# A fused attention and two-layer feed-forward kernel on one core: the up projections recast as Strassen block products

## Time and profile before

| | |
|---|---|
| median of 3 runs | 982.44 us (980.26 to 982.64) |
| the profiled execution | 981.53 us |
| its span in the trace | 979.7 us, mean granted TensorE clock 0.993 |
| PE busy | 956.1 us, 98% |
| DVE, ACT, POOL busy | 49%, 22%, 20% |

### The profile page before, as it was taken

How to read it: one execution, slowest core, us unless ns; L and a number is a source line. 1 busy time by engine, 2 the same in 40 slices (tenths; PEclk the granted TensorE clock), 3 DMA queues, 4 the chain that set the end, 5 groups by cost and what they waited for, 6 DMA issues and landing times.

```text
span 979.7 us, 14496 instructions
## 1 busy us (share of the span) xinstructions
PE 956.1 (98%) x5292; PEld 907.5 (93%) x5292; DVE 481.3 (49%) x895; ACT 219.0 (22%) x444; POOL 198.2 (20%) x211
## 2 busy tenths in 40 slices
PE   6999899999999999999999989999999999999998
PEld 5998899999999999999999968888888888889997
DVE  6776745634634634544555588343334334334332
ACT  4887642210200210110210011111012112111111
POOL 5679473000000000000028896000000000000000
PEclk9999899999999999999999989999999999999999
DMA  8897152000000000000013231010001001001001
GB/s 247 218 229 189 27 146 65 2 1 1 1 0 0 0 0 0 0 0 0 0 33 87 86 86 55 0 39 0 0 0 39 0 0 39 0 0 40 1 1 37
DMA packets 54065, 40.83 MB, mean 42 GB/s; under 512 B 21264, under 2 KB 44304, under 8 KB 54032
## 3 DMA queue, kind: packets, MB, share of 16 engines
q1 hardware_dynamic: 54032, 40.38, 14.9%
HBM read 35.65 MB, written 4.72 MB: 41 GB/s over the span
## 4 chain that ended last, share of the span: by engine, by line
PE 89%; POOL 3%; issue 3%; DMA 1%; DVE 1%; ACT 1%; SPq 0%; POOLq 0%; DVEq 0%; ACTq 0%
PE bank L558 29%; PE bank L559 29%; PE bank L560 29%; POOL probs L462 1%; DMA q_diag<-in_qT 1%; POOL half_sum L456 1%; PE bank L548 1%; PE bank L526 1%; PE bank L534 1%; DVE x_hi L911 0%; PE bank L554 0%; ACT probs L705 0%; POOL mask L429 0%; PE bank L517 0%; POOL ssum L287 0%
## 5 line engine op out<-in xcount | busy, mean ns | idle before, releaser
L558 PE MATMUL bank<-h_hi,wts 128*128 128x384 f32 (+2 forms) x608 | 216.5, 356 | 0.1
L559 PE MATMUL bank<-h_lo,wts 128*128 128x384 f32 (+2 forms) x608 | 215.6, 355 | 0.0
L560 PE MATMUL bank<-h_hi,wts 128*128 128x384 f32 (+2 forms) x608 | 215.1, 354 | 0.0
L558 PE MATMUL bank<-x_split_sb,wts 128*128 128x384 f32 x576 | 193.5, 336 | 0.0
L560 PE MATMUL bank<-x_split_sb,wts 128*128 128x384 f32 x576 | 193.2, 335 | 0.0
L559 PE MATMUL bank<-x_split_sb,wts 128*128 128x384 f32 x576 | 192.9, 335 | 0.0
L935 DVE TENSOR_TENSOR h_f<-h_f 128x464 f32<-128x464 f32 (+1 forms) x80 | 56.7, 709 | 144.1 <-ACT h_f L763 144.1
L558 PE MATMUL bank<-x_hi,wts 128*128 128x464 f32 (+1 forms) x320 | 120.4, 376 | 4.7 <-DVE x_lo L916 4.6
L558 PEld LDWEIGHTS bank<-h_hi,wts 128*128 128x128 f32 x608 | 114.2, 188 | 7.6 <-DVE h_lo L863 0.4
L559 PEld LDWEIGHTS bank<-h_lo,wts 128*128 128x128 f32 x608 | 114.1, 188 | 7.0
L560 PEld LDWEIGHTS bank<-h_hi,wts 128*128 128x128 f32 x608 | 114.2, 188 | 6.3
(11 more groups left out here) (63 smaller groups left out, 1029.3 us busy)
## 6 DMA issues: line engine op xcount, KB each, us to landing
k_sb<-in_kT SPq DMA_DIRECT2D x16, 288.0 KB, 4.0
q_diag<-in_qT SPq DMA_DIRECT2D x32, 144.0 KB, 4.5
v_odd<-in_v_odd SPq DMA_DIRECT2D x16, 256.0 KB, 2.9
v_even<-in_v_even SPq DMA_DIRECT2D x16, 256.0 KB, 3.2
raw<-in_w_in SPq DMA_DIRECT2D x16, 256.0 KB, 2.7
raw<-in_w_down SPq DMA_DIRECT2D x16, 256.0 KB, 2.6
out_T<-acts SPq DMA_DIRECT2D x16, 232.0 KB, 2.0
raw<-in_w_gate SPq DMA_DIRECT2D x12, 256.0 KB, 3.2
```

Source lines behind the costliest of these rows:

```text
L558: pe.matmul(ps, w_hi, v_hi, start=first, stop=False)
L559: pe.matmul(ps, w_hi, v_lo, start=False, stop=False)
L560: return pe.matmul(ps, w_lo, v_hi, start=False, stop=last)
```

## The change

**Shape of the work.** Tokens are taken in 3 pairs of 384-token tiles (768 tokens). There are six runs: the first layer for each pair, then the second layer for each pair. A run first does all its up products and keeps the hidden activations `h` in SBUF (up to 16 x 768 x 4 bytes per partition), then all its down products, chunk by chunk, for both halves of the pair.

**Up products.** A step takes a 2 by 2 arrangement: two blocks of 128 output features (gate and value of one chunk in the first layer, two chunks in the second), two halves of the 512 input features, two tiles of the pair. In place of 8 block products it makes 7 (`p1` to `p7`, Strassen's scheme in Winograd's form), each of 6 matmuls of 384 columns, on sums of weight blocks (S1 to S4) and sums of input blocks (T1 to T4). There are 12 steps in a run of the first layer, 8 in one of the second. PE's order in step u is p1, p7, p3 of step u-1, p6, p2, p4, p5.

**What goes with it.** The split weights are no longer kept: SP streams the raw weights for every run (three DMAs, 512 KB, a step; `load_w`), into two buffers in turn. POOL makes the four weight sums of step u+2 (`weight_sums`, 256 elements a partition each), ACT rounds 1024 and 768 elements a partition (`high1`, `high2`), DVE makes the rests of both (`low1`, `low2`). ACT copies three partial results out of PSUM (`c_t`, `c_p7`, `c_u`), DVE adds the others to them (c11, c21, c22), ACT, DVE and POOL form h from them (`gate_a`, `gate_b`, `silu_a`, `silu_b`, `h_a`, `h_b`; in the second layer ReLU and squares). The sums of squares for the next pair are seven POOL operations of 768 elements, in steps 1 to 7 of the first two runs. In the down part of a run each chunk has 24 matmuls; ACT rounds its weights and h (`down_high` 512 elements, `h_high` 768), POOL and DVE make the rests (`down_low`, `h_low`), and the input blocks of the next run are summed and split (four sums of 768 on DVE, seven roundings on ACT, seven rests on DVE), beginning at chunk 5 of a gated run that is followed by another and at chunk 1 otherwise; the first two steps' weight sums of the next run are made in chunks 2 and 3.

**Attention.** Its loops over batches are written out. The rounding of first-layer weights leaves it; two steps' weight sums, 14 sums of squares of 384 elements in groups 18 to 24 and 28 to 34, two mean squares with root and reciprocal (near groups 28 and 38), eight normalisings, and the blocks of the first pair (from group 34 on) come into it. The first up product follows the last slot.

The diff, cut to its core (a line of "..." marks what is left out):

```diff
+PW = 2 * NT
+PAIRS = TOKENS // PW
...
+UP_STEPS = [C1] * PAIRS + [C2 // 2] * PAIRS
+CHUNKS = [C1] * PAIRS + [C2] * PAIRS
+RUNS = 2 * PAIRS
+U0 = [sum(UP_STEPS[:n]) for n in range(RUNS + 1)]
+M0 = [sum(CHUNKS[:n]) for n in range(RUNS + 1)]
+B_BANKS = (3, 2, 0, 1)
...
+    def load_w(u):
+        if u >= 2:
+            sp.wait_ge(lo1_done, u - 1)
+            sp.wait_ge(lo2_done, u - 1)
+        r = max(n for n in range(RUNS) if U0[n] <= u)
+        s = u - U0[r]
+        one, two_ = ((w_gate, s), (w_val, s)) if first_layer(r) else ((w_in, 2 * s), (w_in, 2 * s + 1))
+        rows = [w.rearrange("(k p) f -> p k f", p=P)[:, :, n * P:(n + 1) * P] for w, n in (one, two_)]
+        to = w_in_sem[u % 2]
+        sp.dma_start(raw_part(u, RAW_A11, 2).rearrange("p (k f) -> p k f", k=KT), rows[0]).then_inc(to, 16)
+        sp.dma_start(two(raw_part(u, RAW_A21)), rows[1][:, 0:2, :]).then_inc(to, 16)
+        sp.dma_start(two(raw_part(u, RAW_A22)), rows[1][:, 2:4, :]).then_inc(to, 16)
...
+    for r in range(RUNS):
+        for u in range(U0[r] + (2 if r == 0 else 3), U0[r + 1] + 2):
+            if u < U0[RUNS]:
+                load_w(u)
+        for m in range(M0[r] + 2, M0[r + 1] + 2):
+            if m < M0[RUNS]:
+                load_d(m)
+        if r + 1 < RUNS:
+            load_w(U0[r + 1] + 2)
+        if not first_layer(r):
+            store(r, 0)
+            store(r, 1)
...
+    def weight_sum(u, i):
+        if i == 0:
+            pool.wait_ge(w_in_sem[u % 2], 48 * (u // 2 + 1))
+            nc.gpsimd.tensor_tensor(raw_part(u, RAW_S1), raw_part(u, RAW_A21), raw_part(u, RAW_A22),
+                                    ALU.add).then_inc(s_add, 1)
+        if i == 1:
+            nc.gpsimd.tensor_tensor(raw_part(u, RAW_S3), raw_part(u, RAW_A11), raw_part(u, RAW_A21),
+                                    ALU.subtract).then_inc(s_add, 1)
+        if i == 2:
+            pool.wait_ge(s_add, 4 * u + 1)
+            nc.gpsimd.tensor_tensor(raw_part(u, RAW_S2), raw_part(u, RAW_S1), raw_part(u, RAW_A11),
+                                    ALU.subtract).then_inc(s_add, 1)
+        if i == 3:
+            pool.wait_ge(s_add, 4 * u + 3)
+            nc.gpsimd.tensor_tensor(raw_part(u, RAW_S4), raw_part(u, RAW_A12), raw_part(u, RAW_S2),
+                                    ALU.subtract).then_inc(s_add, 1)
+    def weight_sums(u):
...
+    def h_a(u, r):
+        n = u - U0[r]
+        if first_layer(r):
+            pool.wait_ge(silu_a_done, u + 1)
+            pool.wait_ge(c21_done, u + 1)
+            nc.gpsimd.tensor_tensor(h_half(n, 0), ga[:], va[:], ALU.mult).then_inc(ha_done, 1)
...
+    def h_b(u, r):
+        n = u - U0[r]
+        if first_layer(r):
+            pool.wait_ge(silu_b_done, u + 1)
+            pool.wait_ge(c22_done, u + 1)
+            nc.gpsimd.tensor_tensor(h_half(n, 1), sbuf_b[:], vb[:], ALU.mult).then_inc(hb_done, 1)
...
+    for r in range(RUNS):
+        for u in range(U0[r], U0[r + 1]):
+            s = u - U0[r]
+            if s >= 1:
+                h_a(u - 1, r)
+            if u + 2 < U0[r + 1]:
+                weight_sums(u + 2)
+            if s >= 1:
+                h_b(u - 1, r)
+            if r + 1 < PAIRS and 1 <= s <= SQ_STEPS:
+                if s == 1 and r == 0:
+                    pool.wait_ge(o_out, 2 * GROUPS)
+                if s == 1 and r > 0:
+                    pool.wait_ge(norm_done, 2 * KT + KT * r)
+                square_step(nc.gpsimd, s - 1, lambda k: pair_cols(r + 1, k), sq1[:], ssum1[:], sq1_step,
+                            SQ_STEPS * r)
+            if u == U0[r + 1] - 1:
+                down_low(M0[r])
+        for m in range(M0[r], M0[r + 1]):
+            f = m - M0[r]
+            if m + 1 < M0[r + 1]:
+                down_low(m + 1)
+            if f == 0:
+                h_a(U0[r + 1] - 1, r)
+                h_b(U0[r + 1] - 1, r)
+            if f in (2, 3) and r + 1 < RUNS:
+                weight_sums(U0[r + 1] + f - 2)
...
+    def product(ps, u, a, b, first):
+        for k in range(2):
+            w = slice(a * HALF_K + k * P, a * HALF_K + (k + 1) * P)
+            x = slice(b * PW + k * NT, b * PW + (k + 1) * NT)
+            mm = three(ps[:, 0:NT], w_hi[u % 2][:, w], w_lo[u % 2][:, w], xc_hi[:, x], xc_lo[:, x],
+                       first and k == 0, k == 1, not first)
+        return mm
...
+    def p3(u, r):
+        x_ready(u, r, X_B22)
+        pe.wait_ge(c22_done, u + 1)
+        product(u_banks(r)[(u - U0[r]) % 2], u, W_S4, X_B22, False).then_inc(p3_done, 1)
...
+    for r in range(RUNS):
+        for u in range(U0[r], U0[r + 1]):
+            s = u - U0[r]
+            p1(u, r)
+            p7(u, r)
+            if s >= 1:
+                p3(u - 1, r)
+            p6(u, r)
+            p2(u, r)
+            p4(u, r)
+            p5(u, r)
...
+        for m in range(M0[r], M0[r + 1]):
+            down(m, r, 0)
+            if m == M0[r]:
+                p3(U0[r + 1] - 1, r)
+            down(m, r, 1)
...
+    def gate_b(u, r):
+        x = u_banks(r)[(u - U0[r]) % 2][:, 0:NT]
+        act.wait_ge(p3_done, u + 1)
+        act.wait_ge(hb_done, u)
+        nc.scalar.activation(sbuf_b[:], x, ACT.Sigmoid if first_layer(r) else ACT.Relu).then_inc(act_b_done, 1)
...
+            act.wait_ge(p1_done, u + 1)
+            if s == 0:
+                act.wait_ge(x_split, 7 * r + X_T1 + 1)
             else:
+                act.wait_ge(c11_done, u)
+            copy(c_t[:], X[s % 2][:, 0:NT], t_out)
+            act.wait_ge(p7_done, u + 1)
+            if s >= 1:
+                act.wait_ge(c22_done, u)
+            copy(c_p7[:], Y[:, 0:NT], p7_out)
+            if u + 1 < U0[r + 1]:
+                high1(u + 1)
             else:
+                down_high(M0[r])
+                h_high(M0[r], r)
+            if s >= 1:
+                gate_b(u - 1, r)
+            act.wait_ge(p6_done, u + 1)
+            if s >= 1:
+                act.wait_ge(c21_done, u)
+            copy(c_u[:], X[s % 2][:, 0:NT], u_out)
+            gate_a(u, r)
+            if u + 1 < U0[r + 1]:
+                high2(u + 1)
...
+    def low2(u):
+        dve.wait_ge(hi2_done, u + 1)
+        nc.vector.tensor_tensor(w_lo[u % 2][:, G1:G1 + G2], w_raw[u % 2][:, HALF_K + G1:HALF_K + G1 + G2],
+                                w_hi[u % 2][:, G1:G1 + G2].bitcast(F32), ALU.subtract).then_inc(lo2_done, 1)
...
+        for u in range(U0[r], U0[r + 1]):
+            s = u - U0[r]
+            if u + 1 < U0[r + 1]:
+                low1(u + 1)
             else:
+                h_low(M0[r])
+            if s >= 1 and first_layer(r):
+                silu_b(u - 1, r)
+            dve.wait_ge(p2_done, u + 1)
+            dve.wait_ge(t_out, u + 1)
+            if s >= 1:
+                if first_layer(r):
+                    dve.wait_ge(ha_done, u)
+                else:
+                    dve.wait_ge(act_a_done, u)
+            nc.vector.tensor_tensor(ga[:], Z[:, 0:NT], c_t[:], ALU.add).then_inc(c11_done, 1)
+            dve.wait_ge(p4_done, u + 1)
+            dve.wait_ge(u_out, u + 1)
+            if s >= 1 and not first_layer(r):
+                dve.wait_ge(h21_done, u - U0[PAIRS])
+            nc.vector.tensor_tensor(va[:], Y[:, 0:NT], c_u[:], ALU.add).then_inc(c21_done, 1)
+            if first_layer(r):
+                dve.wait_ge(act_a_done, u + 1)
+                dve.wait_ge(c11_done, u + 1)
+                nc.vector.tensor_tensor(ga[:], ga[:], sa[:], ALU.mult).then_inc(silu_a_done, 1)
             else:
+                dve.wait_ge(c21_done, u + 1)
+                square(h_half(2 * s + 1, 0), va[:], h21_done)
+            dve.wait_ge(p5_done, u + 1)
+            dve.wait_ge(p7_out, u + 1)
+            if s >= 1:
+                if first_layer(r):
+                    dve.wait_ge(hb_done, u)
+                else:
+                    dve.wait_ge(h22_done, u - U0[PAIRS])
+            nc.vector.tensor_tensor(vb[:], X[s % 2][:, 0:NT], c_p7[:], ALU.add).then_inc(c22_done, 1)
+            if not first_layer(r):
+                dve.wait_ge(c22_done, u + 1)
+                square(h_half(2 * s + 1, 1), vb[:], h22_done)
+            if u + 1 < U0[r + 1]:
+                low2(u + 1)
...
```

More of the change, by code:

```diff
@@ L142, in build @@
[L142 to L158, removed]
@@ L242, in past @@
-        def past(n):
-            return n + START
-        def start(engine, which):
-            for s in starts[which]:
-                engine.sem_inc(s, START)
-        def x_tile(t, k):
-            return acts[:, bass.ds(t * NT + k * TOKENS, NT)]
-        def x2_tile(t, k, cols):
-            return acts[:, bass.ds(t * NT2 + k * TOKENS, cols)]
-        def pieces1(f):
-            return [(wts[:, bass.ds(f * W1 + 2 * n * D, D)], wts[:, bass.ds(f * W1 + (2 * n + 1) * D, D)])
-                    for n in range(3)]
@@ L279, in square_step, with chunk_done @@
+        def chunk_done(engine, m):
+            r = max(n for n in range(RUNS) if M0[n] <= m)
+            if m == M0[r + 1] - 1:
```

(41 more changed lines are left out.)

1115 lines of the change are left out of this document (549 added, 566 removed).

## The result

| | before | changed |
|---|---|---|
| median | 982.12 us (980.26 to 982.64) | 1039.41 us (1037.62 to 1044.13) |
| ratio, 95% interval | | 1.0594 (1.0556 to 1.0633) |
| span of the profiled execution | 979.7 us | 1038.3 us |
| mean granted clock | 0.993 | 0.967 |

The change makes the kernel 5.9% slower. The forecast was slower too, at 998, with a range that ended at 1034; the measured time lies 5 us above it. The three terms of the loss (the loop of the gated steps, the down chunks, attention) were all larger than I took them, and the largest part of attention's, a wait for a load, I had not seen.

The account below looks back on a forecast made before the run. PE, busy 956.1 of 979.7 us, was taken to bound the kernel, paying for columns. 979.7 - 60.0 - 8.5 + 3 + 73 + 9 = 996.2, plus 1.8 outside the span: 998.0 us, range 952 to 1034.

Parts of the forecast that it names:

- Columns: Layer matmuls: 4536 of 384 columns, 790.2 us, in place of 850.2 us before; -60.0 us.
- the turn of the layers: Between first and second layer: next blocks made under down chunks, so PE's waits and half clock go; -8.5 us.
- The squared steps: Second layer's up steps: c22 does not wait for h_b, and the chain ends before it is wanted; 0 (to +5).
- The loop: Gated layer: chain of c22, low2, SP, load, weight sums, h_b, next c22 outlasts PE's 7.32 us step; +73 us.
- walks: Passes once round the gated layer's chain, one per step; 27 over three runs, the first of each counted.
- T: Length of one walk of the gated layer's chain: 10.5 us with a square step, 9.8 without.
- X: End of h_b(u-1) on POOL in the gated layer, from which the chain's times are counted.
- Down chunks: Down parts: POOL's sums against DVE's two-input work, 3 us at each of three turns before squared runs; +9 us (0 to 18).
- Attention: Attention: squares +3, roots and reciprocals +4, drain -2, fewer DMAs -2; +3 us (-3 to +8).
- Hidden after all: Rival, gated steps: load and sums fit inside 7.32 us and PE stays full; 925 us, chance 0.05.
- the loop, but short: Rival, gated steps: load 3.1, sums 0.55, no port wait, T 8.3; 948 us, chance 0.17.
- The third rival: Gated steps and turns: POOL too waits out DVE's two-input work, 1018 us; with clock falls 1038; chance 0.2.

Follow-up runs that it names:

- run 0: No follow-up: the changed kernel's first of six runs, first (gated) layer, first pair; 10.72 us a step, steps 1 to 9.
- run 2: No follow-up: the changed kernel's third of six runs, first (gated) layer, third pair, without squares; 10.13 us a step, steps 1 to 9.
- the run with late loads: Against the changed kernel, only attention's first two weight loads (i 8, 9 for 1, 2) and their sums (groups 36 to 43) moved later; 1030.4 us.

## Why the prediction was wrong, point by point

- **Columns** (-60.0) and **the turn of the layers** (-8.5): right. 174.2 ns a matmul; no gap before the squared layer. The last run, which prepares no other, goes from c22 of step 0 at 916.18 to the start of PE's last matmul at 1034.92; with the 0.17 of that matmul and 6.6 us ahead of that c22 (as in run 0, from 129.6 to 136.18) it is 125.5, against 8 x 7.32 + 16 x 4.18 = 125.4. The squared steps (0) were right too, 7.36 us each.
- **The loop** (+73): the mechanism, its members and its walks were right, the size was 84. T was 10.4 in the mean over the walks of runs 0 and 1 and 9.8 in run 2, measured 10.7 and 10.1. What was mis-sized is the load: from SP's first issue to POOL's first sum the 24 walks took 3.8 to 4.8 us, 4.27 in the mean, for my 3.6 + 0.1. SP's later issues took 0.5 each, not 0.37, which is some 0.2 of it; the rest is in the transfers and stays open. The other members took 0.3 less than I had: `low2` ended 2.2 or 2.6 after X with squares (2.55) and 1.8 without (1.85), SP began 0.07 behind it (0.15), and sums with `h_b` took 3.85 to 4.25 (4.1). The rest is the entry: step 1 came 10.5 to 11.4 after step 0, which I had at 10.0.
- **Down chunks** (+9): the step that failed in size, and in half of its argument. From c22 to c22 the runs last 172.8, 173.8, 171.2, 131.1 and 131.1 us; less the work of PE (138.0 or 125.4, and in the first two runs 1.3 for the matmuls that sum the squares over the features) and the loop there remain 4.1, 5.2, 7.8, 5.7 and 5.7, together 28.5. For the three turns to a squared run I had said 3 each; they are 5.7 to 7.8, of which PE's waits for `d_lo` are 3.6 to 5.8. For the other two I had said "no chunk is late", because DVE's reciprocals have one input. They have; but in DVE's chunks 3 and 4 four normalisings, with two inputs, meet the second set of sums (263.97 to 269.65 in run 0), and PE waits 2.9 us. The prediction has no word on these normalisings.
- **Attention** (+3, with 8 as its upper end): the step that failed outright. It cost 15.8, and attention ended past the 125 us that I had named as a sign of being wrong. I priced squares, roots, the drain and fewer DMAs, and never asked when the loads of the weight sums arrive: they are issued behind q, k and v on an SP that itself waits for groups to finish. By the run with late loads they cost, with the sums and roundings that stand on them, 10.7 us by group 17, a term that the sum does not have. The squares and the first root, 5 in the sum, cost 7.2; the second root and the drain, 0 in the sum, 0.3; what left attention gave 2.4 where nothing stood in it, for my 2. My own rule, to follow each added wait to what stands behind it, was applied in the layers and not in attention.
- **Sum.** 11 + 19.5 + 12.8 more than predicted make 996.2 into 1039.5; the trace has 1038.3.
- **The rivals.** "Hidden after all" and "the loop, but short" are refuted by the walk itself. The third rival, with 1018 to 1038, came nearest to the time, for partly other reasons. Of the Trainium skill's rule on the shared port ("SBUF — State Buffer", section "Who interferes with whom") the trace now shows both sides: POOL's sum goes from 0.74 to 1.46 beside DVE's two-input work, which it had hardly done in the rows of before. A pair takes 1.41, strict turns would take 1.57, so the second is held up for less than the whole of the first. From "less so for POOL" I had taken that POOL's sums stay near 0.7 us beside DVE, and that does not hold where both engines have a queue.
- **The clock.** Idle spells of up to 3.4 us a step did bring it down, in some steps. Stretches of the changed kernel (columns as the earlier trace rows):

```profile
372.00:373.00 1.00, 0.00 (x0) 0.00 (x0) 0.00 (x0) 0.00 (x0) 1.00 (x2) 1.00 0.00 0
373.00:374.00 1.00, 0.07 (x1) 0.07 (x1) 0.68 (x2) 0.03 (x1) 1.00 (x2) 1.00 0.00 0
...
375.00:376.00 1.00, 1.00 (x5) 1.00 (x4) 0.98 (x2) 0.49 (x2) 1.00 (x1) 0.50 0.00 0
378.00:379.00 1.00, 1.00 (x8) 1.00 (x7) 0.05 (x1) 0.33 (x1) 0.00 (x0) 1.00 0.75 184
```

  PE's p5 still ended before it was needed, and a fall cost the step little. It came in 11 of the 24 walks. In runs 0 and 1 the part from POOL's first sum to the end of `h_b` takes 4.1 to 4.25 us in the eight walks with a fall and 3.85 to 3.87 in the eight without, for 0.3 of which one of the sums is enough that meets a late `silu_a` (L408, 1.05 in place of 0.74, in five of the eight). In run 2 it is 4.2 in three walks with a fall and 3.87 to 4.2 in five without. So the clock is worth some 3 us of the 84. The steps themselves differ by more, since the load varies: c22 to c22 from 362.86 is 10.46 us with full clock and a load of 3.94, from 351.97 and 373.32 it is 10.89 and 11.09 with a fall and loads of 4.32 and 4.57. The clock was not varied by itself.
- **Range.** It ended at 1034, though my own third rival went to 1038. It was meant to hold the bounds of the unknown costs, but was built from one chain's spread. The errors of three terms had the same sign, because each was a wait of POOL or for POOL, and I treated them as independent.

## What to carry to other kernels

When a change moves work to an engine that had been idle, shares of busy time say little: write down, for every operation that waits for a DMA, what stands behind it on its queue and who waits for that, and add up each closed chain through buffers, loads and engines against the period of the bottleneck. Do it for every stage that the change touches, the prologue too, and ask of each load when its issuer reaches it. If a chain is longer than the period, look for one order or one buffer that opens it before anything is made faster: here two exchanged lines were worth 67 us.

## What the runs showed of the hardware that I had not expected

- Two queues of two-input work, POOL's sums of 256 elements and DVE's operations on 768, fall into step: one of each in 1.41 us, where alone they follow each other after 0.69 and 0.88. POOL's operation takes twice its time alone (1.46 for 0.74), DVE's one and a half times (1.50 for 0.95).
- In `load_w` SP took 0.37 us for the first DMA issue and 0.51 and 0.47 for the two right behind it. Whether it is the place or the other shape of these two was not tried.
- PE stood before p3 for 0.6 to 3.35 us in each step of 10 to 11. The clock fell in 11 of 24 such steps: the waits there were 2.2 to 3.35, in the others 0.6 to 3.1. In the 50 us stretches that hold mostly such steps the granted clock was 0.88 to 0.97.
